# Attention on one core: TensorE takes two pipeline steps as one, and ScalarE takes its exponential ahead of its copy

## The reference, cut to what matters

```python
batch, n_heads, seq, head_dim = (4, 8, 576, 64)
scores = scale * np.matmul(q, k.transpose(0, 1, 3, 2))
thresh = np.max(scores, axis=-1, keepdims=True) - tau
scores = np.where(scores >= thresh, scores, -1000000000.0)
scores = scores - np.max(scores, axis=-1, keepdims=True)
attn = np.exp(scores)
attn = attn / (np.sum(attn, axis=-1, keepdims=True) + 1e-09)
attn_out = np.matmul(attn, v)
# heads side by side: x is 2304 tokens x 512; then two layers, g = h - tanh(h) and g = h * sigmoid(h)
h = x @ w_in        # 512 x 2048
x = g @ w_out       # 2048 x 512
```

## Time and profile before

| | |
|---|---|
| time, median of 3 runs | 1015.45 us (1014.68 to 1015.56) |
| the profiled execution | 1016.35 us, its span 1014.5 us |
| busy over the whole span | TensorE matmul 991.1 us (98%), VectorE 830.2 (82%), ScalarE 715.9 (71%), GpSimd 462.4 (46%) |
| TensorE's granted clock | full in all 40 slices |
| score matmuls | 672 in 144 groups, the first at 5.9 us, the last at 287.3 |
| transposes | 656 |
| value product records | 640, the last at 300.5 us |
| first matmul of the layers | 300.85 us |

### The profile page before, as it was taken

One profiled execution on the slowest core, in us unless ns is written; L12 is line 12 of the kernel. 1 busy time (PEld: TensorE's weight loads), 2 busy tenths in 40 slices (PEclk: granted clock), 3 DMA queues, 4 the chain that ended last, 5 costly groups with the idle time before them and its releaser, 6 DMA issues.

```text
span 1014.5 us, 18094 instructions
## 1 busy us (share of the span) xinstructions
PE 991.1 (98%) x6002; PEld 900.0 (89%) x6002; DVE 830.2 (82%) x1633; ACT 715.9 (71%) x1441; POOL 462.4 (46%) x509
## 2 busy tenths in 40 slices
PE   6999999999999999999999999999999999999998
PEld 5666667776769999999999999999999999999998
DVE  8999999999988899598996989776894559935675
ACT  6999999999977765577646757387654676457642
POOL 5999999999967420264004540074201450024000
PEclk9999999999999999999999999999999999999999
DMA  6244454634212858437783567538675247734286
GB/s 217 77 174 158 175 188 142 225 110 164 97 49 101 291 192 254 157 115 259 224 252 107 197 220 247 174 118 292 197 253 172 64 169 238 237 125 166 78 253 210
DMA packets 57867, 181.00 MB, mean 178 GB/s; under 512 B 5040, under 2 KB 6576, under 8 KB 57776
## 3 DMA queue, kind: packets, MB, share of 16 engines
q1 hardware_dynamic: 57488, 179.78, 53.0%
q10 hardware_dynamic: 288, 0.07, 0.0%
HBM read 145.75 MB, written 34.08 MB: 177 GB/s over the span
## 4 chain that ended last, share of the span: by engine, by line
PE 86%; DVE 5%; DMA 3%; issue 2%; ACT 1%; POOL 1%; SPq 0%; ACTq 0%; DVEq 0%; POOLq 0%
PE b L1393 31%; PE b L1311 28%; PE scores L1272 10%; PE pv L1235 10%; PE tps L1294 7%; DMA w_raw<-w_in 3%; DVE g_op L1132 1%; DVE w_op L1043 1%; DVE x_sum L1066 1%; DVE c L1118 1%; POOL w_sum L566 1%; DVE c L1101 0%; DVE b L1086 0%; ACT b L838 0%; DVE stage L1051 0%
## 5 line engine op out<-in xcount | busy, mean ns | idle before, releaser
L1311 PE MATMUL b<-x_op,w_op 128*128 128x384 f32 x2016 | 355.4, 335 | 5.1 <-ACT b L838 5.0
L1311 PEld LDWEIGHTS b<-x_op,w_op 128*128 128x128 f32 x2016 | 349.0, 188 | 9.7 <-ACT b L838 8.6
L1393 PE MATMUL b<-g_op,w 128*128 128x384 f32 x2016 | 352.6, 334 | 0.5 <-DVE g_op L1132 0.5
L1393 PEld LDWEIGHTS b<-g_op,w 128*128 128x128 f32 x2016 | 349.4, 188 | 2.0 <-issue 2.0
L566 POOL TENSOR_TENSOR w_sum<-w_raw 128x256 f32<-128x256 f32 x94 | 75.2, 800 | 260.5 <-DMA w_raw<-w_in 132.1
L975 DVE TENSOR_SCALAR_CACHE_REDUCE probs<-scores,fine 128x576 f32<-128x576 f32 x144 | 116.9, 812 | 12.1 <-PE scores L1272 11.5
L880 ACT ACTIVATE g_op<-c 128x768 fp32r<-128x768 f32 x96 | 81.2, 846 | 61.0 <-DVE c L1118 34.2
L1272 PEld LDWEIGHTS scores<-k_lo,q_parts 128*128 128x128 f32 x336 | 63.8, 193 | 65.1 <-issue 38.3
L1043 DVE TENSOR_TENSOR w_op<-w_sum,w_op 128x512 fp32r<-128x512 f32 x94 | 77.1, 820 | 53.8 <-ACT w_op L793 49.3
L642 POOL TENSOR_SCALAR probs<-probs,rinv 128x576 f32<-128x576 f32 x144 | 109.3, 759 | 19.5 <-DVE rinv L1000 12.7
L1007 DVE SCALAR_TENSOR_TENSOR probs<-scores,stats,probs 128x576 f32<-128x576 f32 x144 | 117.8, 818 | 0.1
(11 more groups left out here) (89 smaller groups left out, 1338.1 us busy)
## 6 DMA issues: line engine op xcount, KB each, us to landing
w<-scr SPq DMA_DIRECT2D x168, 512.0 KB, 4.5
w_raw<-w_in SPq DMA_DIRECT2D x56, 512.0 KB, 3.8
scr<-w_op SPq DMA_DIRECT2D x8, 1792.0 KB, 8.5
scr<-stage SPq DMA_DIRECT2D x8, 1792.0 KB, 8.4
k_raw<-k_in SPq DMA_DIRECT2D x15, 576.0 KB, 5.8
q_raw<-q_in SPq DMA_DIRECT2D x15, 576.0 KB, 8.0
v_all<-v_in SPq DMA_DIRECT2D x16, 320.0 KB, 3.2
stage_raw<-w_in SPq DMA_DIRECT2D x8, 512.0 KB, 4.2
```

The lines of the kernel that those rows point to most:

```text
L1311: last = pe.matmul(out, a, b, start=fresh and k == 0 and i == 0, stop=k == 1 and i == 2, skip_group_check=True)
L1393: last = pe.matmul(bank[n][kind], x, y, start=fresh and q == 0 and f == 0 and i == 0, stop=q == 3 and f == 1 and i == 2, skip_group_check= ...
```

## The change

TensorE's loop over steps takes two at a time, k even and k + 1: the scores of both, then the transposes of both, then what product falls on k. For that the product is cut in other pieces, all of which begin at even k. A pair that begins at an even step (the first table of `L_PV`) has chunks 2, 3 and 2, 2, 1; one that begins at an odd step 2, 3 and 2, 3. The output copies move by a step for the even ones. ScalarE's exponential stands ahead of the copies of its step. Nothing is computed otherwise; VectorE, GpSimd and SyncE have the same lists.

```diff
-L_PV = {L_T + 8: (0, 0, 1), L_T + 9: (0, 1, 2), L_T + 10: (0, 2, 3), L_T + 11: (0, 3, 5),
-        L_T + 12: (1, 0, 1), L_T + 13: (1, 1, 2), L_T + 14: (1, 2, 3), L_T + 15: (1, 3, 5)}
-L_OUT = {L_T + 12: 0, L_T + 16: 1}
+L_PV = ({L_T + 7: (0, 0, 2), L_T + 9: (0, 2, 5), L_T + 11: (1, 0, 2), L_T + 13: (1, 2, 4), L_T + 15: (1, 4, 5)},
+        {L_T + 8: (0, 0, 2), L_T + 10: (0, 2, 5), L_T + 12: (1, 0, 2), L_T + 14: (1, 2, 5)})
+L_OUT = {L_T + 11: 0, L_T + 17: 1}, {L_T + 12: 0, L_T + 16: 1}
 ...
         # ScalarE, in each step
+                    q = k - L_EXP
+                    if here(q):
+                        ...
+                        act.wait_ge(lift_done, n + 1)
+                        act.activation(tile, tile, ACT.Exp, bias=stats[:, c, 0:1], scale=-SCALE / FINE,
+                                       accum_out=rowsum[:, c:c + 1]).then_inc(exp_done, 1)
                     for kind, q, number in units_of(k - L_T, first):
                         ...
-                    q = k - L_EXP
-                    if here(q):
-                        ...
 ...
         # TensorE
-                for k in ks:
-                    ...
+                for k in ks[::2]:
+                    two = [s for s in (k, k + 1) if s in ks]
+                    for s in two:
+                        scores_of(s)
+                    for s in two:
+                        transposes_of(s)
                     product(k)
```

More of the change, by code:

```diff
@@ L49 @@
 VCOLS = (FULL + 1) * P
-L_PV = {L_T + 8: (0, 0, 1), L_T + 9: (0, 1, 2), L_T + 10: (0, 2, 3), L_T + 11: (0, 3, 5),
-        L_T + 12: (1, 0, 1), L_T + 13: (1, 1, 2), L_T + 14: (1, 2, 3), L_T + 15: (1, 3, 5)}
-L_OUT = {L_T + 12: 0, L_T + 16: 1}
-TAIL = (PAIRS - 1) * TILES + max(L_OUT) + 1
+L_PV = ({L_T + 7: (0, 0, 2), L_T + 9: (0, 2, 5), L_T + 11: (1, 0, 2), L_T + 13: (1, 2, 4), L_T + 15: (1, 4, 5)},
+        {L_T + 8: (0, 0, 2), L_T + 10: (0, 2, 5), L_T + 12: (1, 0, 2), L_T + 14: (1, 2, 5)})
+L_OUT = {L_T + 11: 0, L_T + 17: 1}, {L_T + 12: 0, L_T + 16: 1}
+TAIL = (PAIRS - 1) * TILES + max(L_OUT[1]) + 1
 SKIP_AT = 4
@@ L715, in steps @@
                 for k in ks:
-                    for lag, a in L_OUT.items():
+                    for parity, lag, a in ((i, lag, a) for i in range(2) for lag, a in L_OUT[i].items()):
                         q = k - lag
-                        if q % TILES == 0 and here(q):
+                        if q % TILES == 0 and q // TILES % 2 == parity and here(q):
                             p, i = q // TILES, 2 * (PAIRS * B + q // TILES) + a
@@ L724, in steps @@
                             last.then_inc(out_taken, 1)
+                    q = k - L_EXP
+                    if here(q):
+                        n, c, tile = STEPS * B + q, q % RING, probs[:, slot_of(q), :]
+                        act.wait_ge(lift_done, n + 1)
+                        act.activation(tile, tile, ACT.Exp, bias=stats[:, c, 0:1], scale=-SCALE / FINE,
+                                       accum_out=rowsum[:, c:c + 1]).then_inc(exp_done, 1)
                     for kind, q, number in units_of(k - L_T, first):
@@ L1208, in product @@
                 def product(k):
-                    for lag, (a, i0, i1) in L_PV.items():
+                    for lag, (a, i0, i1) in (*L_PV[0].items(), *L_PV[1].items()):
                         q = k - lag
@@ L1238, in product, with scores_of @@
                                 last.then_inc(pv_done, 1)
-                for k in ks:
+                def scores_of(k):
                     q = k - L_S
@@ L1274, in steps, with transposes_of @@
                         last.then_inc(scores_done, 1)
+                def transposes_of(k):
                     for kind, q, number in units_of(k - L_T, first):
```

## The result

The changed kernel took 1020.47 us (median of 6 runs, 1019.62 to 1023.03), the kernel before 1015.48 in the runs beside it (1014.68 to 1017.88). The ratio is 1.0054, with a 95% interval of 1.0041 to 1.0067: slower by 0.5%, as forecast, and the forecast of 1019.5 is 1 us off. The profiled executions stand 1020.33 against 1016.35, their spans 1018.4 against 1014.5.

What follows compares the result with a forecast made beforehand. TensorE was taken as the bound, by a little. Seven rounds' idle time of 19.2 us, less 15.9 lost now, plus 0.75 early gave +4.0 us: 1019.5 us, forecast 1017.5 to 1023 (chance 0.53), range 1012.5 to 1025.5.

Steps and rivals of the forecast that it cites:

- What is added: a wait with work behind it: TensorE's second score group waits for VectorE's second pass, transposes and product behind it; 2.75 us idle per 18 tiles.
- A: Run of tiles 0,1 in two pairs, 8 transposes and 2 chunks: VectorE idles 0.23 us ahead of it.
- C: Run of tiles 4,5, 9 transposes and 2 chunks: VectorE idles 0.05 us ahead of it.
- D: Run of tiles 6,7, 8 transposes and 3 chunks, tile 8 next: VectorE idles 0.15 us ahead of it.
- E: Run of tile 8 and the next pair's tile 0, 8 transposes, 2 chunks: VectorE idles 1.05 us ahead of it.
- G: Run of the second pair's tiles 3,4, 12 transposes and 2 chunks: VectorE idles 0.58 us ahead of it.
- I: Run of the second pair's tiles 7,8, ten matmuls in its second score group: VectorE idles 0.69 us ahead of it.
- ScalarE's new order: Exponential ahead of the copies of its step: put at no cost, with 9.5 us as the upper end.
- the rival of a late ScalarE: Copies behind exponentials keep TensorE waiting: 1029 us, from half of it on 1024; chance 0.13.
- Rival 1: Transposes pass the held score group, so TensorE's waits cost nothing and 15.9 us go: 999.5 us; chance 0.15 for faster.
- Rival 2: Transposes plus product of a run take 0.15 us less than worked out, saving 5 us: 1015 us; chance 0.17.
- The clock: Rival: TensorE's clock falls, score matmuls stand 0.24 us apart, 55 us more, over 1070 us; chance 0.02.

Runs made afterwards that it cites:

- before_half: The kernel before, with GpSimd scaling only the first 288 of 576 columns of each probability tile; ratio 0.9993 to the kernel before.
- exp_alone: The kernel before, with only ScalarE's exponential moved ahead of the copies of its step; ratio 0.9982 to the kernel before.
- stst: The changed kernel, with TensorE's order in two steps scores, transposes, scores, transposes, product; ratio 0.9968 to the kernel before.
- chunk_early: The changed kernel, with one chunk of odd pairs' first half moved from the run ahead of tile 8 to the run before; ratio 1.0028 to the kernel before.

## Why the prediction was right

- **What bounds the kernel.** TensorE, by a little: held up by before_half (GpSimd relieved, no gain) and exp_alone (two of four product stalls less from 50 to 275 us, 1.1 us, and 0.2% gained).
- **What is added: a wait with work behind it.** Shown three ways: by the trace (161.42, 1.98 behind VectorE's start), by stst, which takes the transposes out from behind the wait and turns +0.54% into -0.32%, and by chunk_early. By the prediction's letters, forecast and measured idle times in the steady rounds are A 0.23 and 0.24, C 0.05 and 0.05, D 0.15 and 0.16, E 1.05 and 1.05, G 0.58 and 0.59, I 0.69 and 0.70: 2.75 and 2.79 in all.
- **The sum.** From tile 17 to 143 VectorE took 252.31 us (39.80 to 292.11), 3.9 over before; up to tile 17 0.5 more; the end of attention 13.03 instead of 13.19. Together 4.3 where 4.0 was forecast; 0.4 came back in the layers. The ratio says 5.5 (4.2 to 6.8) and the medians differ by 5.0, so the single profiled pair may be a little low.
- **The second score group where it isn't held** was put at 0.53, a choice between 0.45 and 0.63. It is 0.53 in tile 85, behind tile 84's group, in matmuls 0.13 apart from the first on:

```profile
173.86 0.29 PE L1271 MATMUL scores<-k_lo,q_parts 128*128 128x288 f32 x1
173.99 0.29 PE L1271 MATMUL scores<-k_hi,q_parts 128*128 128x288 f32 x1
...
174.39 1.47 PE L1294 MATMUL tps<-ident,probs 128*128 128x128 f32 x12
```

  Behind tile 8's ten matmuls it is 0.61 (165.90 to 166.51), and those ten take 1.26 where 1.31 was put. So TensorE's 32.6 us hold within 0.1. That VectorE's idle time ahead of the next round's tile 0 came as forecast rests on this term.
- **Hold mis-sized, without effect:** TensorE was to be idle for at most 0.44 us before a second group. That holds where the first group comes just in time. Behind tile 8 TensorE is early: tile 82's scores start at 168.60, 0.35 before VectorE would need them (169.88 - 0.93), and tile 83's are held by 0.79 instead of 0.44, of which the row shows 0.62:

```profile
170.02 0.40 PE L1271 MATMUL scores<-k_lo,q_parts 128*128 128x288 f32 x1 [0.62 <-DVE probs L1007]
```

  It costs nothing, since the added hold is time that TensorE had to spare. The longest such wait is 1.1 us, in the first round.
- **ScalarE's new order at nothing:** right in its number, wrong in its weight. From 50 to 275 us no product waits any more (two do at the end of attention, 0.49 and 0.69 us), and the rival of a late ScalarE was refuted by the 0.2 us above; that the old order would have made the change cost 2% was foreseen nowhere.
- **Rival 1, the hold does not hold:** refuted by the same rows. Its price, 999.5, also left GpSimd out, which at stst's pace already costs 3.8 us; whether it would have stopped the gain there, no run shows.
- **Rival 2, no change, because T + P is shorter:** refuted. Eight transposes take 0.96 us, twelve 1.40, and the products 0.63, 1.12 and 1.61, within 0.01 of what was put. Only the eight behind tile 17's ten score matmuls take 1.02, and those ten, unheld, 1.16 where 1.21 was put, so the two cancel.
- **The clock:** the granted clock reads full throughout, and four score matmuls take 0.63 to 0.65 us behind every hold from tile 7 on. As before, they stand 0.24 us apart for the first 18 us, though it reads full there too.

## What to carry to other kernels

Grouping instructions on an in-order engine moves every wait of the group ahead of all that stood between its members. Before grouping, write down for each wait what now stands behind it, from the wait to the next thing the other engine needs, and compare that with the time the other engine leaves; the sum of busy times shows nothing of it. And when four engines are nearly all the time busy, price a gain by the second bound before believing it: leaving out half the work of one engine shows in one run whether it is next.

## What was not expected of the hardware

What a group of score matmuls costs depends on what stands right ahead of it. Behind a product, or behind a hold, the second record comes 0.23 to 0.25 us after the first; behind eight transposes 0.22 (171.87 to 172.09 before). Behind another ordinary score group it comes after 0.13 (173.86 to 173.99), as within a group: there the start costs nothing, and a group of four takes 0.53 instead of 0.63 us. But behind the ten matmuls of tile 8 it is 0.21 again (165.90 to 166.11), in all seven rounds; why, no run shows.
